# A long two-stage kernel: ten ahead units instead of eight, seven of them in three passes, and late weights loaded one by one

## The chip, the cores and the metric

The kernel runs on one core of a Trainium2 chip. The metric is the device time of one execution in microseconds (us), lower is better. Five things work side by side on the core: TensorE (PE, its weight loads are listed as PEld), VectorE (DVE), ScalarE (ACT), GpSimd (POOL) and the DMA queues, which SyncE (SP) and here and there ACT issue. A program counts its hand-overs with semaphores, and each engine runs its own list in order, so an instruction that waits holds up all that stands behind it on its engine.

## The reference

```python
def _attn_ref(x, filt_r, filt_i):            # x: 2 x 3008 x 256
    X = np.fft.rfft(x, axis=1)
    Y = X * (filt_r + 1j * filt_i)[None, :, :]
    return np.fft.irfft(Y, n=x.shape[1], axis=1).astype(np.float32)

def _moe_ref(x, w_in, w_out, alpha):         # 6016 x 256, w_in 256 x 2048, w_out 2048 x 256
    h = x @ w_in
    g = np.maximum(h, 0.0) + alpha * np.minimum(h, 0.0)
    return (g @ w_out).astype(np.float32)

def _moe2_ref(x, w_in, w_out):
    h = np.maximum(x @ w_in, 0.0)
    return (h * h @ w_out).astype(np.float32)

def reference(**kwargs):
    x = _attn_ref(x, filt_r, filt_i).reshape(B * S, D)
    return _moe2_ref(_moe_ref(x, ...), ...)
```

## The kernel before

**Spectral part.** Each batch element ("first" = b0, "second" = b1) is transformed as a 47 x 64 Fourier transform, all as matrix products. For the second element the first stage is 16 units (`A_UNITS`) of 96 x 512 numbers. One unit is one matmul with the 96 x 96 matrix `const_a1`, a copy of its PSUM bank to SBUF by ACT, and a store to the DRAM tensor `t_rows` by SP. Operands in plain fp32 make two matmul records per unit. Where operands are split in a high and a low part, both of type fp32r, a product is three matmuls, high x high, low x high and high x low, one record each; the feed-forward layers and the spectra of the first element work in that way.

**Slots.** After the first element's spectral part come 192 slots, n = 0 to 191: 12 groups of some 500 tokens, each through 8 pairs of weight tiles p = 0 to 7, for each of the two layers. `up(n)` is 12 matmuls; ACT (`L757`) and DVE (`L945`, `L955`) make the hidden pieces from them; POOL makes two more sums of pieces (`L621` and `L624`, named T2 and T4); ACT rounds seven pieces to `g_hi` (`L633`), DVE forms `g_lo` (`L930`), and two slots later PE does `down_high(n - 2)` (14 matmuls, `L1188` and `L1190`) and `down_low(n - 2)` (7 matmuls, `L1201`). In slots 0 and 1 there is no down part.

**Weights.** A weight pair p is loaded by SP to `w_raw`, four sums of its tiles are made (by five POOL instructions, `L563` to `L569`, for p = 0 to 4, and by four DVE instructions, `L846` to `L853`, for p = 5 to 7, which is `LATE_W` on), ACT rounds it to `w_hi`, and POOL subtracts to `w_lo` (`L553`). `up(p)` of the first group waits for `w_lo`. Pairs 5 to 7 are late because their place in SBUF holds `a_ahead` and `x_ahead` first, the results and inputs of the ahead units.

**Ahead units.** Eight units (`AHEAD_A`) of the second element run before slot 0 (`transform_ahead`, `L1029`): unit 0 before the last inverse of the first element, units 1 to 5 after `y_first(0)`, units 6 and 7 after `y_first(1)`. `y_first(half)` (`L1112`) makes half of group 0 from `vc`, which is the stored result `v_rows` of the first element loaded again. The other eight units (`transform_1`, `L1035`) stand behind slots 0, 1, 2, 2, 3, 3, 4, 4 (`A_SLOT`). SP stores the ahead results two units at a time (`store_ahead`), and loads weight pairs 5, 6 and 7 in one go when all eight are stored (`a_ahead_stored`).

The order on every engine is written out by hand: the blocks `@block.sync`, `@block.gpsimd`, `@block.scalar`, `@block.vector` and `@block.tensor` are the lists of SP, POOL, ACT, DVE and PE.

Of the kernel before, what the change touches and what calls it, by code (L numbers as in the profile page):

```python
# [1383 lines left out]
```

## Time and profile before

| | us |
|---|---|
| median of three runs | 1112.49 |
| lowest and highest | 1112.28, 1113.65 |
| the profiled execution, its own time | 1113.78 |
| span of its instructions | 1112.0 |

The profile page divides the span by engine. PE is busy for 1105.1 us of the span, DVE for 961.0, ACT for 663.8, POOL for 643.8. The busy time of PE is modelled and its matmuls are pipelined, so the start of one matmul and that of the next tell more than the length of either. The chain of work that ended last, followed backwards from the last instruction, is 86% PE. The granted TensorE clock is 1.00 of full speed over the whole span, 2.4 GHz.

### The profile page before, as it was taken

The page shows a single profiled execution, that of the slowest core. Times are in us where ns is not written, and L with a number is a line of the kernel's source. Part 1 is how long each engine was busy: PE and PEld are TensorE (multiplying, and loading weights), DVE is VectorE, ACT ScalarE, POOL GpSimd, SP SyncE. Part 2 cuts the span into 40 slices and gives each one's busy share as a digit, 9 for nine tenths or more (in the row PEclk, how much of TensorE's full clock was granted, in tenths as well). Part 3 has the DMA queues.
Part 4 walks back from the last instruction along what each step waited for, and adds up shares of the span by engine and source line. Part 5 has one row for each costly group of instructions (what it writes and reads, how often), then busy time and mean ns, then how long its engine had stood idle before and what let it go on. Part 6 is the DMA issues. An engine that isn't in the chain of part 4 may idle for free.

```text
span 1112.0 us, 17235 instructions
## 1 busy us (share of the span) xinstructions
PE 1105.1 (99%) x6911; PEld 985.3 (89%) x6911; DVE 961.0 (86%) x1100; ACT 663.8 (60%) x785; POOL 643.8 (58%) x479
## 2 busy tenths in 40 slices
PE   8999999999999999999999999999999999999998
PEld 7568989898999999999999999999999999999998
DVE  4758999999898988888888898888888888888887
ACT  5966667666556555655556656555555555555654
POOL 1836687877566556556557455555555555455453
PEclk9999999999999999999999999999999999999999
DMA  9973325152130421221218510110110110110100
GB/s 251 271 212 88 93 77 155 47 156 61 40 114 1 139 88 52 88 88 52 88 64 314 210 38 1 38 38 1 38 38 1 38 38 1 38 37 1 38 19 20
DMA packets 57865, 88.22 MB, mean 79 GB/s; under 512 B 4920, under 2 KB 45624, under 8 KB 57784
## 3 DMA queue, kind: packets, MB, share of 16 engines
q1 hardware_dynamic: 57584, 86.95, 25.3%
q8 instruction: 55, 0.90, 0.3%
q14 instruction: 26, 0.21, 0.1%
q10 hardware_dynamic: 200, 0.15, 0.0%
HBM read 53.79 MB, written 33.29 MB: 78 GB/s over the span
## 4 chain that ended last, share of the span: by engine, by line
PE 86%; DVE 5%; POOL 3%; issue 2%; ACT 2%; DMA 1%; SPq 0%; ACTq 0%; DVEq 0%; POOLq 0%
PE bank L1156 14%; PE bank L1161 14%; PE bank L1157 14%; PE bank L1190 12%; PE bank L1188 12%; PE bank L1201 12%; PE bank L1133 2%; DVE y_im_b L836 1%; DVE g_lo L930 1%; ACT swapped_b L633 1%; PE bank L1002 1%; DVE g_raw L945 1%; PE bank L1056 1%; PE bank L1058 1%; POOL g_raw L621 1%
## 5 line engine op out<-in xcount | busy, mean ns | idle before, releaser
L621 POOL TENSOR_TENSOR g_raw<-g_raw 128x250 f32<-128x250 f32 (+1 forms) x191 | 272.1, 1425 | 391.8 <-DVE g_raw L955 391.8
L930 DVE TENSOR_TENSOR g_lo<-g_raw,g_hi 128x1750 fp32r<-128x1750 f32 (+1 forms) x191 | 424.6, 2223 | 49.6 <-ACT g_hi L633 48.7
L757 ACT ACTIVATE g_raw<-bank 128x500 f32<-128x500 f32 (+1 forms) x384 | 226.1, 591 | 316.2 <-PE bank L1161 275.7
L633 ACT ACTIVATE g_hi<-g_raw 128x1750 fp32r<-128x1750 f32 (+1 forms) x191 | 318.9, 1670 | 56.9 <-POOL g_raw L624 54.9
L1190 PE MATMUL bank<-g_hi,w_lo 128*128 128x250 f32 (+1 forms) x1337 | 320.2, 279 | 0.0
L1188 PE MATMUL bank<-g_hi,w_hi 128*128 128x250 f32 (+1 forms) x1337 | 319.8, 279 | 0.0
L1156 PE MATMUL bank<-in_hi,w_hi 128*128 128x500 f32 (+1 forms) x768 | 302.3, 394 | 0.0
L1157 PE MATMUL bank<-in_hi,w_lo 128*128 128x500 f32 (+1 forms) x768 | 298.3, 388 | 0.0
L1190 PEld LDWEIGHTS bank<-g_hi,w_lo 128*128 128x128 f32 x1337 | 252.7, 189 | 7.5
L1188 PEld LDWEIGHTS bank<-g_hi,w_hi 128*128 128x128 f32 x1337 | 252.5, 189 | 7.5
L624 POOL TENSOR_TENSOR g_raw<-g_raw 128x250 f32<-128x250 f32 (+1 forms) x191 | 244.7, 1281 | 15.0
L1161 PE MATMUL bank<-in_lo,w_hi 128*128 128x500 f32 (+1 forms) x768 | 236.8, 390 | 0.0
L1201 PE MATMUL bank<-g_lo,w_hi 128*128 128x250 f32 (+1 forms) x1337 | 187.7, 279 | 0.0
L1201 PEld LDWEIGHTS bank<-g_lo,w_hi 128*128 128x128 f32 x1337 | 171.5, 189 | 2.5 <-DVE g_lo L930 0.7
L1161 PEld LDWEIGHTS bank<-in_lo,w_hi 128*128 128x128 f32 x768 | 144.4, 188 | 30.1
L1156 PEld LDWEIGHTS bank<-in_hi,w_hi 128*128 128x128 f32 x768 | 144.6, 188 | 24.4 <-issue 1.6
L1157 PEld LDWEIGHTS bank<-in_hi,w_lo 128*128 128x128 f32 x768 | 144.5, 188 | 23.6 <-issue 1.4
L945 DVE SCALAR_TENSOR_TENSOR g_raw<-g_raw,rest_sb,bank 128x500 f32<-128x500 f32 (+1 forms) x192 | 136.2, 730 | 25.4 <-ACT g_raw L757 25.1
L948 DVE TENSOR_TENSOR g_raw<-g_raw,bank 128x500 f32<-128x500 f32 (+1 forms) x192 | 127.6, 671 | 32.3 <-ACT g_raw L757 31.3
L955 DVE TENSOR_TENSOR g_raw<-g_raw 128x500 f32<-128x500 f32 (+1 forms) x192 | 136.7, 712 | 6.6
L553 POOL TENSOR_TENSOR s_lo<-s_raw,s_hi 128x512 fp32r<-128x512 f32 (+1 forms) x24 | 32.9, 1371 | 1.4 <-DVE in_lo L886 1.4
L553 POOL TENSOR_TENSOR w_lo<-w_raw,w_hi 128x1408 fp32r<-128x1408 f32 x8 | 26.4, 3305 | 7.0 <-ACT w_hi L633 7.0
(91 smaller groups left out, 611.2 us busy)
## 6 DMA issues: line engine op xcount, KB each, us to landing
filt_b<-filt SPq DMA_DIRECT2D x36, 256.0 KB, 4.7
v_rows<-v_out_b SPq DMA_DIRECT2D x24, 256.0 KB, 3.5
vc<-v_rows SPq DMA_DIRECT2D x22, 256.0 KB
w_rows<-s_hi SPq DMA_DIRECT2D x8, 704.0 KB, 3.7
w_rows<-s_lo SPq DMA_DIRECT2D x8, 704.0 KB, 3.2
w_hi<-w_rows SPq DMA_DIRECT2D x8, 704.0 KB, 5.2
w_lo<-w_rows SPq DMA_DIRECT2D x8, 704.0 KB, 7.7
w_raw<-w SPq DMA_DIRECT2D x8, 512.0 KB, 6.1
```

The source lines that it names most:

```text
L621: pool.tensor_tensor(g_raw[:, r, T2, 0:h], g_raw[:, r, B22, 0:h], g_raw[:, r, T1N, 0:h], ALU.add).then_inc(t2_ready, 1)
L624: pool.tensor_tensor(g_raw[:, r, T4, 0:h], g_raw[:, r, B21, 0:h], g_raw[:, r, T2, 0:h], ALU.subtract).then_inc(t4_ready, 1)
L633: return act.activation(dst, src, ACT.Copy)
L757: act.activation(g_raw[:, r, 2 * j:2 * j + 2, 0:h], h_ps[j][:, 0:2 * h].rearrange("p (j d) -> p j d", j=2), ACT.Relu, scale=-1.0 if n < SL ...
L930: dve.tensor_tensor(g_lo[:, q, B11:T4 + 1, 0:h], g_raw[:, q, B11:T4 + 1, 0:h], g_hi[:, q, :, 0:h], ALU.subtract).then_inc(g_lo_ready, 1)
L945: dve.scalar_tensor_tensor(out=piece, in0=piece, scalar=rest_sb[:, f:f + 1], in1=hidden, op0=ALU.mult, op1=ALU.add).then_inc(g_ready, 1)
L1156: pe.matmul(o, w_hi[:, p, 2 * j + k, :], in_hi[:, g % 2, k, cols], start=(k == 0), stop=False)
L1157: pe.matmul(o, w_lo[:, p, 2 * j + k, :], in_hi[:, g % 2, k, cols], start=False, stop=False)
L1161: mm = pe.matmul(o, w_hi[:, p, 2 * j + k, :], in_lo[:, g % 2, k, cols], start=False, stop=(k == KD - 1))
L1188: pe.matmul(o, w_hi[:, p, tile, :], g_hi[:, q, piece - B11, 0:h], start=(first and (side == 0 or g == LAST_G and b == 3)), stop=False, ski ...
L1190: pe.matmul(o, w_lo[:, p, tile, :], g_hi[:, q, piece - B11, 0:h], start=False, stop=False, skip_group_check=True)
L1201: mm = pe.matmul(o, w_hi[:, p, tile, :], g_lo[:, q, piece, 0:h], start=False, stop=(last or final and b < 3), skip_group_check=True)
```

## The change

Ten units run ahead instead of eight, and six stay behind slots: 0, 1, 2, 2, 3, 3. Unit 0 stays as it was. Units 1 to 7 all stand between `y_first(0)` and `y_first(1)` and go in three passes: `x_ahead` is rounded to `x_hi` (units 1 and 2 by POOL, 3 to 7 by ACT), DVE subtracts in place to `x_lo`, and the matrix comes in split form too (`a1_parts`, cast by POOL from a `const_a1` load that is three times as wide). Units 8 and 9 are in plain fp32 after `y_first(1)`, from the ordinary buffers `x_raw`. Two more PSUM banks, 4 and 5, take ahead units, and so `up(0)` waits for the copy of unit 5. SP issues the loads of units 8 and 9 ahead of the last store of `v_rows`. Weight pair 5 is loaded as soon as the first four ahead units are stored, 6 and 7 after the rest, and the sums of pair 5 move from DVE in slot 2 to POOL ahead of slot 0; those of pairs 6 and 7 are on DVE in slots 2 and 3 instead of 3 and 4.

```diff
-AHEAD_BANK = (2, 3, 0, 1)
-AHEAD_PART = (1, AHEAD_A - 2, AHEAD_A)
-A_SLOT = [None] * AHEAD_A + [0, 1, 2, 2, 3, 3, 4, 4]
+AHEAD_ALL = AHEAD_A + 2
+AHEAD_BANK = (2, 3, 0, 1, 4, 5)
+AHEAD_PART = (1, AHEAD_A, AHEAD_ALL)
+A_SLOT = [None] * AHEAD_ALL + [0, 1, 2, 2, 3, 3]
...
+LATE_SUMS = LATE_W + 1
...
@@ block.sync @@
             for n in range(B_UNITS):
+                if n == B_UNITS - 1:
+                    for u in range(AHEAD_A, AHEAD_ALL):
+                        load_x(u)
                 store_v(f0, *divmod(n, B_HALF), n % f0.vs)
...
+            def load_late(p):
+
+                for j in IN_PLACE[p - LATE_W]:
+                    sp.wait_ge(a_ahead_stored[j], 32)
+                load_w1(p)
+
             store_ahead(0)
-            for u in range(AHEAD_A, AHEAD_A + f1.xs):
+            store_ahead(2)
+            for u in range(AHEAD_ALL, AHEAD_A + f1.xs):
                 load_x(u)
-            for u in range(2, AHEAD_A, 2):
-                store_ahead(u)
-            sp.wait_ge(a_ahead_stored, 16 * AHEAD_A)
-            for p in range(LATE_W, FP):
-                load_w1(p)
+            store_ahead(4)
+            load_late(LATE_W)
+            store_ahead(6)
+            for u in range(AHEAD_A, AHEAD_ALL):
+                load_x(u + f1.xs)
+            for u in range(AHEAD_A, AHEAD_ALL):
+                store_t(f1, u, u % f1.outs)
+            for p in range(LATE_W + 1, FP):
+                load_late(p)
@@ block.gpsimd @@
             for p in range(LATE_W):
                 if p + 1 < LATE_W:
                     w_sums(p + 1)
+                else:
+
+                    pool.wait_ge(const_a1_loaded, 16)
+                    pool.tensor_copy(a1_parts[:, :], const_a1_sb[:, ROWS:3 * ROWS]).then_inc(a1_parts_ready, 1)
+                    x_high(1)
+                    x_high(2)
                 w_low(p)
...
             for s in f0.v_stored:
                 pool.wait_ge(s, 16 * (B_UNITS // f0.vs + 1))
+
+            w_sums(LATE_W)
@@ block.scalar @@
+                if n == B_UNITS - 1:
+                    x_high(3)
...
             for u in range(AHEAD_PART[0]):
                 ahead_copy(u)
+            x_high(4)
             v_copy(f0, B_UNITS - 1, (B_UNITS - 1) // f0.vs, (B_UNITS - 1) % f0.vs, (B_UNITS - 1) % 2)
+            x_high(5)
...
             in_high(0, (0,))
+            x_high(6)
+            x_high(7)
             act.wait_ge(f0.v_stored[(B_UNITS - 1) % f0.vs], 48)
@@ block.vector @@
+            for u in range(1, 6):
+                x_low(u)
             in_low(0, (0,))
+            for u in range(6, AHEAD_A):
+                x_low(u)
...
-                if LATE_W <= n + 3 < FP:
-                    w_sums(n + 3)
+                if LATE_SUMS <= n + 4 < FP:
+                    w_sums(n + 4)
@@ block.tensor @@
+                if 0 < u < AHEAD_A:
+                    pe.wait_ge(a1_parts_ready, 1)
+
+                    pe.wait_ge(x_lo_ready, u)
+                    pe.matmul(ps, a1_parts[:, 0:ROWS], x_hi[:, u - 1, :], start=True, stop=False)
+                    pe.matmul(ps, a1_parts[:, ROWS:2 * ROWS], x_hi[:, u - 1, :], start=False, stop=False)
+                    pe.matmul(ps, a1_parts[:, 0:ROWS], x_lo[:, u, :], start=False, stop=True).then_inc(f1.a_done, 1)
+                    return
```

On PE, between the two halves of `y_first`, three rows stood before, of which the middle one is ahead units 1 to 5 (two records each):

```order
L1112 MATMUL bank<-const_y_sb,vc 128x34
L1029 MATMUL bank<-x_ahead,const_a 96x512 x5
L1112 MATMUL bank<-const_y_sb,vc 128x94 x5
L1112 MATMUL bank<-const_y_sb,vc 128x34
L1029 MATMUL bank<-x_ahead,const_a 96x512 x2
L1156 MATMUL bank<-in_hi,w_hi 128x504
```

After the change, the end of that stretch reads (the first three rows here are the last of seven such triples):

```order
L1105 MATMUL bank<-x_hi,a_parts 96x512
L1106 MATMUL bank<-x_hi,a_parts 96x512
L1107 MATMUL bank<-x_lo,a_parts 96x512
L1197 MATMUL bank<-const_y_sb,vc 128x94 x5
L1197 MATMUL bank<-const_y_sb,vc 128x34
L1114 MATMUL bank<-x_raw_b,const_a 96x512 x2
L1241 MATMUL bank<-in_hi,w_hi 128x504
```

Two units in fp32 still stand behind `y_first(1)`, now units 8 and 9, and the seven in three passes all stand ahead of it.

On POOL, the passage from the weights of the first slots to the first T2 and T4 (`L621`, `L624`) was:

```order
L569 TENSOR_TENSOR w_raw<-w_raw 128x128
L553 TENSOR_TENSOR w_lo<-w_raw,w_hi 128x1408 x2
L621 TENSOR_TENSOR g_raw<-g_raw 128x252
L624 TENSOR_TENSOR g_raw<-g_raw 128x252
L621 TENSOR_TENSOR g_raw<-g_raw 128x252
```

and is now:

```order
L588 TENSOR_TENSOR w_lo<-w_raw,w_hi 128x1408
L617 CAST a_parts<-const_a 96x192
L608 CAST x_hi<-x_ahead 96x512 x2
L588 TENSOR_TENSOR w_lo<-w_raw,w_hi 128x1408
L598 TENSOR_TENSOR w_raw<-w_raw 128x128
L600 TENSOR_SCALAR w_raw<-w_raw 128x128
L601 TENSOR_TENSOR w_raw<-w_raw 128x128
L602 TENSOR_TENSOR w_raw<-w_raw 128x128
L604 TENSOR_TENSOR w_raw<-w_raw 128x128
L668 TENSOR_TENSOR g_raw<-g_raw 128x252
L671 TENSOR_TENSOR g_raw<-g_raw 128x252
```

The five rows from `L598` on are the sums of pair 5; they wait for its load, and slot 0's T2 and T4 (`L668`, `L671`) stand behind them.

On SP, with what each waits for, the stores of the ahead units and the late weights stood so:

```order
L339 DMA t_rows<-a_ahead 48x8x128 [waits a_out_ready_b1]
L339 DMA t_rows<-a_ahead 48x8x128
L327 DMA x_raw_b<-x 96x512 x4
L339 DMA t_rows<-a_ahead 48x8x128 [waits a_out_ready_b1]
L339 DMA t_rows<-a_ahead 48x8x128
L339 DMA t_rows<-a_ahead 48x8x128 [waits a_out_ready_b1]
L339 DMA t_rows<-a_ahead 48x8x128
L339 DMA t_rows<-a_ahead 48x8x128 [waits a_out_ready_b1]
L339 DMA t_rows<-a_ahead 48x8x128
L380 DMA w_raw<-w 128x1024 [waits a_ahead_stored]
L380 DMA w_raw<-w 128x1024 x2
```

and now:

```order
L359 DMA t_rows<-a_ahead 48x8x128 [waits a_out_ready_b1]
L359 DMA t_rows<-a_ahead 48x8x128
L359 DMA t_rows<-a_ahead 48x8x128 [waits a_out_ready_b1]
L359 DMA t_rows<-a_ahead 48x8x128
L347 DMA x_raw_b<-x 96x512 x2
L359 DMA t_rows<-a_ahead 48x8x128 [waits a_out_ready_b1]
L359 DMA t_rows<-a_ahead 48x8x128
L400 DMA w_raw<-w 128x1024 [waits a_ahead_stored1,a_ahead_stored0]
L359 DMA t_rows<-a_ahead 48x8x128 [waits a_out_ready_b1]
L359 DMA t_rows<-a_ahead 48x8x128
```

The load of pair 5 (`L400`) now waits for the first two pairs of stores, with the third issued ahead of it and the fourth behind it.

## Rows read from the trace of the kernel before

**Rows 1.** The page: busy time (share) and instructions of PE, and the chain by engine

```profile
PE 1105.1 (99%) x6911; PEld 985.3 (89%) x6911; DVE 961.0 (86%) x1100; ACT 663.8 (60%) x785; POOL 643.8 (58%) x479
...
PE 86%; DVE 5%; POOL 3%; issue 2%; ACT 2%; DMA 1%; SPq 0%; ACTq 0%; DVEq 0%; POOLq 0%
```

**Rows 2.** The chain in order of time, 55 to 80: start us, us, what

```profile
55.99 2.43 DMA v_rows<-v_out_b
...
59.05 2.08 DMA vc<-v_rows
61.26 1.50 PE bank L1112 x12
...
64.53 0.23 PE bank L1156
...
74.48 0.12 PE bank L1188
...
76.12 0.81 PE bank L1201 x7
76.93 1.72 PE bank L1035 x4
```

**Rows 3.** Timeline of PE, 45.1 to 46: start us, us, engine line op tiles shape

```profile
45.14 0.39 PE L1044 MATMUL bank<-t_hi_b,const 128*128 128x512 f32 x1
45.37 0.40 PE L1046 MATMUL bank<-t_lo_b,const 128*128 128x512 f32 x1
45.61 0.59 PE L1056 MATMUL bank<-y_re_b,const_full 128*128 128x512 f32 x1
```

**Rows 4.** Timeline of ACT, 40 to 105

```profile
56.63 0.59 ACT L633 ACTIVATE in_hi<-bank 128x504 fp32r<-128x504 f32 x1 [0.66 <-PE bank L1112]
...
59.34 2.54 ACT L633 ACTIVATE a_ahead<-bank 96x512 f32<-96x512 f32 x5 [2.12 <-PE bank L1029]
...
71.40 1.67 ACT L633 ACTIVATE g_hi<-g_raw 128x1764 fp32r<-128x1764 f32 x1
```

**Rows 5.** Timeline of DVE, 45 to 105

```profile
57.32 0.68 DVE L886 TENSOR_TENSOR in_lo<-bank,in_hi 128x504 fp32r<-128x504 f32 x1 [4.52 <-ACT in_hi L633]
...
72.31 0.69 DVE L955 TENSOR_TENSOR g_raw<-g_raw 128x504 f32<-128x504 f32 x1
73.10 2.56 DVE L930 TENSOR_TENSOR g_lo<-g_raw,g_hi 128x1764 fp32r<-128x1764 f32 x1
...
92.47 0.28 DVE L846 SCALAR_TENSOR_TENSOR w_raw<-w_raw 128x128 f32<-128x128 f32 x1
...
94.38 1.98 DVE L930 TENSOR_TENSOR g_lo<-g_raw,g_hi 128x1764 fp32r<-128x1764 f32 x1
```

**Rows 6.** Timeline of POOL, 20 to 110

```profile
22.58 0.46 POOL L563 TENSOR_TENSOR w_raw<-w_raw 128x128 f32<-128x128 f32 x1 [22.16 <-DMA w_raw<-w]
...
24.57 0.46 POOL L569 TENSOR_TENSOR w_raw<-w_raw 128x128 f32<-128x128 f32 x1
...
69.55 0.74 POOL L621 TENSOR_TENSOR g_raw<-g_raw 128x252 f32<-128x252 f32 x1 [14.78 <-DVE g_raw L955]
70.37 0.73 POOL L624 TENSOR_TENSOR g_raw<-g_raw 128x252 f32<-128x252 f32 x1
...
73.89 2.37 POOL L624 TENSOR_TENSOR g_raw<-g_raw 128x252 f32<-128x252 f32 x1
```

**Rows 7.** Timeline of SP's queue, 0 to 130

```profile
59.96 0.82 SPq L339 DMA_DIRECT2D t_rows<-a_ahead  x2
```

**Rows 8.** Tile a_ahead: the eight stores of SP, issue to landing

```profile
DMA to landing us min/median/max: 2.6/3.7/4.1
```

**Rows 9.** Tile w_raw, 55 to 110: the three late loads, issue to landing

```profile
DMA to landing us min/median/max: 3.6/4.5/6.6
```

**Rows 10.** Busy times of 61 to 70.5; the last number is GB/s moved

```profile
61.00:70.50 9.50, 9.33 (x43) 6.78 (x43) 3.18 (x5) 5.04 (x9) 0.87 (x2) 1.00 0.90 245
```

**Rows 11.** Timeline of PE, 96.6 to 97.4

```profile
96.71 0.86 PE L1201 MATMUL bank<-g_lo,w_hi 128*128 128x252 f32 x6
```

More of the change, by code:

```diff
@@ L92 @@
 LATE_W = 5
+LATE_SUMS = LATE_W + 1
+IN_PLACE = [range(p * W_T * P // (2 * COLS), min(AHEAD_A // 2, -(-(p + 1) * W_T * P // (2 * COLS))))
+            for p in range(FP - LATE_W)]
 W2_SLOT = [38, 45, 51, 58, 66, 74, 82, 90]
 W2_LOW = ((3, 0, 4), (4, 4, 8), (5, 8, W_T))
+X_PLACE = 17 * P
 WARM_COLS, WARM_X = 2 * P, 3
@@ L282, in spectral_mix_two_ffn @@
         x_ahead_loaded = [sem(f"x_ahead_loaded{n}") for n in range(AHEAD_A // 2)]
-        a_ahead_stored = sem("a_ahead_stored")
+        a_ahead_stored = [sem(f"a_ahead_stored{n}") for n in range(AHEAD_A // 2)]
+        a1_parts_ready = sem("a1_parts_ready")
+        x_hi_pool, x_hi_act, x_lo_ready = sem("x_hi_pool"), sem("x_hi_act"), sem("x_lo_ready")
         y_done = sem("y_done")
@@ L469, in _ @@
                 if n < SLOTS_1:
-                    for u in range(AHEAD_A, A_UNITS):
+                    for u in range(AHEAD_ALL, A_UNITS):
                         if A_SLOT[u] == n and u + f1.xs < A_UNITS:
                             load_x(u + f1.xs)
-                    for u in range(AHEAD_A, A_UNITS):
+                    for u in range(AHEAD_ALL, A_UNITS):
                         if A_SLOT[u] + 1 == n:
@@ L481, in _ @@
                             if u == 0:
-                                sp.wait_ge(a_ahead_stored, 16 * AHEAD_A)
+                                for stored in a_ahead_stored:
+                                    sp.wait_ge(stored, 32)
                                 for s in f1.a_stored:
@@ L677, in ahead_copy, with x_high @@
                 act.wait_ge(f1.a_done, done(u))
-                copy(a_ahead[:, u, :], m_ps[AHEAD_BANK[u % 4]][0:ROWS, :]).then_inc(f1.a_out_ready, 1)
+                copy(a_ahead[:, u, :] if u < AHEAD_A else f1.a_out[:, u % f1.outs, :],
+                     bank[AHEAD_BANK[u % len(AHEAD_BANK)]][0:ROWS, :]).then_inc(f1.a_out_ready, 1)
+            def x_high(u):
+                act.wait_ge(x_ahead_loaded[u // 2], 16)
+                copy(x_hi[:, u - 1, :], x_ahead[:, u, :]).then_inc(x_hi_act, 1)
             for u in range(0, TURN_UNIT, 2):
@@ L733, in _ @@
                 if n < SLOTS_1:
-                    for u in range(AHEAD_A, A_UNITS):
+                    for u in range(AHEAD_ALL, A_UNITS):
                         if A_SLOT[u] + 1 == n:
@@ L855, in w_sums @@
             def w_sums(p):
-                sums(w_raw[:, p, :, :], w_loaded[p], 16, (w_sums_ready, w_sum_step), p - LATE_W)
+                sums(w_raw[:, p, :, :], w_loaded[p], 16, (w_sums_ready, w_sum_step), p - LATE_SUMS)
             def t_low(n):
@@ L887, in in_low, with x_low @@
                                       in_hi[:, g % 2, half, 0:2 * HALF[k]], ALU.subtract).then_inc(in_lo_ready, 1)
+            def x_low(u):
+                if u < 3:
+                    dve.wait_ge(x_hi_pool, u)
+                else:
+                    dve.wait_ge(x_hi_act, u - 2)
+                dve.tensor_tensor(x_lo[:, u, :], x_ahead[:, u, :], x_hi[:, u - 1, :], ALU.subtract
+                                  ).then_inc(x_lo_ready, 1)
+            for u in range(1, 6):
+                x_low(u)
             in_low(0, (0,))
+            for u in range(6, AHEAD_A):
+                x_low(u)
             for s in f0.v_stored:
@@ L1214, in _ @@
             pe.wait_ge(f0.v_ready, done(B_UNITS - 1))
+            pe.wait_ge(f1.a_out_ready, done(len(AHEAD_BANK) - 1))
             for n in range(2 * SLOTS_1):
@@ L1218, in _ @@
                 if n == LAG:
-                    pe.wait_ge(f1.a_out_ready, done(AHEAD_A - 1))
+                    pe.wait_ge(f1.a_out_ready, done(AHEAD_ALL - 1))
                 if n >= LAG:
@@ L1232, in _ @@
                     ys = sum(FP * k + Y_P < n for k in range(GROUPS - 1))
-                    for u in range(AHEAD_A, A_UNITS):
+                    for u in range(AHEAD_ALL, A_UNITS):
                         if A_SLOT[u] == n:
```

51 lines of the change are left out of this document (34 added, 17 removed).

## The prediction, made before the changed kernel ran

> **What bounds the kernel now.** I read the page first, for the share of each engine and the chain by engine [rows 1]. PE is busy for 99% of the span and carries 86% of the chain; no other engine carries more than 5%. So a microsecond of matmul that disappears is a microsecond of time, unless a wait takes its place, and a wait that is added on PE costs its full length. Next I read the chain in order of time over the stretch that is changed [rows 2], to get the moments at which PE reaches each step: the last store of v_rows is issued at 55.99 and lands at 58.42, the reloaded vc arrives at 61.1, y_first(1) begins at 61.26, slot 0 at 64.53, down_high(0) at 74.48, down_low(0) at 76.12, and two fp32 units behind a slot take 1.72. Then I read the timelines of the other engines over the same stretch, to see how long before each of these moments its inputs are ready [rows 4 to 7], and the landing times and the rate of the DMAs [rows 8 to 10].
>
> **Three passes instead of fp32.** A fp32 unit costs 1.72 / 2 = 0.86 us of PE [rows 2]. Three passes over 512 columns are not in the trace on 96 rows, but they are on 128: successive starts are 0.23 and 0.24 apart [rows 3], so one unit is 3 x 0.235 = 0.70 us. Seven units save 7 x 0.16 = 1.1 us.
>
> **The order around y_first(1).** y_first(0) is done at 56.57, just before ACT's copy starts at 56.63 [rows 4]. Before, five units follow: 56.57 + 5 x 0.86 = 60.87, and PE stands idle until 61.26, 0.39 us. Now seven short units follow: 56.57 + 7 x 0.705 = 61.50. vc is there by then, so y_first(1) begins 0.24 later than before, and since two fp32 units still follow, slot 0 does too. Behind slot 4 two units of 0.86 are gone. Ahead of any new wait the sum is +0.24 - 1.72 = **-1.48 us**, of which 1.1 is the cheaper product and 0.39 the idle time filled.
>
> **Preparing the operands.** This I cost at nothing, and the cover is idle time. ACT's five roundings of 512 columns take a pitch of 0.49 us each (five copies in 2.54, [rows 4]). It has 0.66 idle before 56.63 and 2.12 before 59.34, and the two roundings that stand in the latter take 1.0; the other three stand at steps where it waits for PE. DVE's x_low are 512 columns wide, like its 0.68 us in_low, and it stands idle for 4.52 us before 57.32 [rows 5]; five of them take about 3.1 and the last two come after 57.9, while PE needs unit 6 at 60.1. POOL's two casts of 512 columns and one of 192 have no row; twice its 0.74 for 252 columns gives 1.5 each, some 3.6 in all, before a w_lo that slot 4 first needs. POOL does nothing at all for 14.78 us before 69.55 [rows 6]. If this cover failed, each 1 us of lateness in x_lo would delay PE by up to 1 us. ACT's copies of units 1 to 5 run from 59.34 to 61.88, ahead of the moments at which units 7, 8 and 9 and slot 0 need their banks.
>
> **Loads ahead of the last v_rows store.** Units 8 and 9 bring 0.39 MB that now stands ahead of that store. At 245 GB/s [rows 10] it occupies the queue for 1.6 us. SP issues it when the store before has been issued, so most of it should be through before 57, when the data of the store at 55.99 begins to move. I take 0; the upper bound is 1.6 less PE's new slack of 0.4, 1.2 us.
>
> **The sums of pair 5.** Here the change adds a wait. POOL's five sums wait for the load of pair 5, and behind them on POOL are T2(0) and T4(0); behind T4(0) ACT's g_hi(0), behind it DVE's g_lo(0), and PE's down(0) needs both. Let L be the landing of that load. The sums take 22.58 to 25.03, 2.45 us [rows 6], T2 and T4 from 69.55 to 71.10, 1.55, g_hi 1.68 [rows 4], g_lo 1.98 when alone [rows 5]; with four hand-overs of about 0.06 that is L + 7.9. PE now wants g_lo(0) at 76.12 + 0.24 = 76.36. So the wait is free up to L = 68.5, and above that PE loses L - 68.5.
>
> When is L? SP may issue the load when the first four units are stored. The copy of unit 3 ends at 59.34 + 0.59 + 2 x 0.49 = 60.9 [rows 4]; SP is free then (it ends its first two stores at 60.78, [rows 7]), so the second two stores are issued at 60.95 and 61.4. Stores land 2.6 to 4.1 after issue, the median is 3.7 [rows 8], so the load is issued between 64.0 and 65.5, likely at 65.0. A late load took 3.6 when the queue was empty and up to 6.6 behind others [rows 9]. That bounds L by 64.0 + 3.6 = 67.6 and 65.5 + 6.6 = 72.1. To choose, I count bytes from 61.0, when the data of the first store begins to move: six stores and two x loads of 0.197 MB, and 0.524 MB of weights, 2.1 MB in all. At 245 GB/s this takes 8.6 us, and a landing comes about 0.4 after the last byte: 70.0. With an empty queue it would be 65.0 + 3.6 = 68.6. Between the two I take L = 69.5, nearer to the count, since four DMAs do stand in the queue ahead of this load, and the new wait as 69.5 - 68.5 = **+1.0 us**.
>
> **POOL against DVE.** T4 took 0.73 alone but 2.37 at 73.89, while g_lo was running on DVE [rows 5, 6]: one engine holds the other up. With L = 69.5, T2(0) and T4(0) fall on 72.0 to 73.6, where DVE has its L955 of 0.69 at 72.31. Neither may touch the other, or T4(0) may come 0.7 later; the bounds are 0 and +0.7. I take **+0.2**, as a short overlap is nearer to the short row. The Trainium skill, page "SBUF — State Buffer", section "SBUF: two separate sides", says that a DVE instruction with two SBUF inputs and a GpSimd instruction share one port pair as an exclusive lock, held for the whole instruction by whichever starts first. By that rule the full 0.7 falls due and the sum ends at +0.2 instead of -0.3; the row at 73.89 agrees with it in kind.
>
> **Late weights otherwise.** Before, DVE makes pair 7's sums from 92.47 to 94.38 and g_lo(3) after them, done at 96.36, while PE starts down_low(3) at 96.71 [rows 5, 11]. With two units gone PE would want it at 96.71 - 1.48 = 95.2, a stall of 1.1. But DVE's sums are gone from slot 4, which is 1.9 us, and that leaves 0.8 to spare. So this edit gives no time itself; it keeps the 1.72 from being given back.
>
> **The sum.** -1.48 + 1.0 + 0.2 = **-0.3 us**. The profiled execution (1113.78, span 1112.0) would be at 1113.5, and since the median of the runs shown is 1.29 less than the profiled one, I forecast a median of 1112.49 - 0.3 = **1112.2 us**. A measurement of this kernel can tell some 0.2% from no change, 2.2 us; this forecast is "the same".
>
> **Rivals.**
> 1. **The load of pair 5 is early.** If L is 68.5 or less, POOL is never late and the whole -1.48 stays: 1111.0. For it: an empty queue gives 67.6 to 69.1. Against: two x loads and two stores are in the queue ahead of it. The Trainium skill, page "DMA: Bandwidth & Descriptors", section "Anatomy of one DMA — SWDGE (gpsimd) path", fits one DMA by a fixed 2.0 us and its bytes at 436 GB/s; that makes 3.2 us for this load and so this case, against 3.6 in the emptiest row here.
> 2. **The load of pair 5 is late, and the kernel slower.** The mechanism is the same chain on POOL, and it turns the sign from L = 69.8 on. At L = 71 the stall is 2.5, and -1.48 + 2.5 + 0.2 = +1.2 gives 1113.7; at the bound of 72.1 it is 3.6, and with the contention at 0.2 or 0.7 the net is +2.3 or +2.8: 1114.8 to 1115.3. The largest landing times in the rows speak for it; against it, that 6.6 belongs to a load with two others of its size ahead.
> 3. **The vc path is late.** The two x loads push the last store back by up to the bound of 1.2: 1112.2 + 1.2 = 1113.4. ACT's copies of units 1 to 5 stand behind that store too.
> 4. **The change doesn't bring its gain**, because the x_lo aren't there when PE is, or three passes on 96 rows are no cheaper than fp32: then 1.1 is missing: 1113.3.
>
> **Chances.** The forecast case (L from 68.6 to 70.3) 50%, rival 1 20%, rival 2 18%, rivals 3 and 4 5% each, and 2% for something faster than all of this. For 8 in 10 the range goes from 1110.8, the full gain with the usual scatter of the runs, to 1114.0, rival 2 up to L of 71.3. The chance of faster by over 0.2% (below 1110.3) is 0.04, since no case gives it without scatter; slower by over 0.2% (above 1114.7) needs rival 2 near its bound or with rival 3, 0.07; within, 0.89, which holds nearly all of every case.
>
> **What would show it.** In the profile after: triples on PE with starts 0.235 apart and y_first(1) at 61.5 without idle; POOL's first sum with an idle time ended by the DMA of w_raw, near 69.5, and T2(0) near 72 instead of 69.55; PE idle, or in the chain DVE's g_lo, ahead of down_low(0) at about 77.5; slot 5's down_low(3) at about 96.4 instead of 96.71. The forecast is wrong if POOL's first sum starts before 68.5 or after 70.5, or if a wait shows anywhere else on PE before slot 8.

## The result, and the profile after

The changed kernel takes 1120.09 us (median of 6 runs, 1118.78 to 1120.61) against 1113.62 for the kernel before on the same chip (6 runs, 1112.28 to 1114.29): a ratio of 1.0059, interval 1.0046 to 1.0072. It is slower by 0.6%, where -0.3 us was forecast; the range ended at 1114.0. The profiled execution took 1119.06, with a span of 1117.1, so it is 5.3 us above the profiled one of before, and its span is 5.1 longer.

From the profile page after, the same two rows as in [rows 1]: busy time by engine, then the chain by engine.

```profile
PE 1106.6 (99%) x6918; PEld 988.1 (88%) x6918; DVE 971.9 (87%) x1103; ACT 666.8 (60%) x790; POOL 646.8 (58%) x487
...
PE 83%; DVE 6%; POOL 4%; issue 2%; ACT 2%; DMA 2%; SPq 1%; ACTq 0%; DVEq 0%; POOLq 0%
```

PE fell from 86% to 83% of the chain, and DVE, POOL and DMA rose by a point each. To see where, I cut both traces where the first product with `w_lo` of each slot starts (us, worked out from the starts of PE's rows; "to slot 0" is counted from the last inverse of the first element, since the start-up before it scatters):

| kernel | to slot 0 | 0 to 2 | 2 to 3 | 3 to 4 | 4 to 5 | 5 to 6 | 0 to 6 | 6 to 40 |
|---|---|---|---|---|---|---|---|---|
| before | 10.71 | 7.20 | 6.93 | 6.92 | 6.92 | 7.52 | 35.49 | 203.70 |
| after | 10.73 | 7.20 | 9.80 | 10.20 | 5.79 | 7.54 | 40.53 | 203.74 |

All of the 5 us lies in slots 2, 3 and 4: +2.9 and +3.3 in two of them, and in slot 4 only 1.1 is gained where two units are gone that took 1.72 together. From slot 6 on nothing differs. PE's waits between 55 and 106, all that there are (engine, tile and line waiting, what released it, us in total, times, longest):

```profile
PE bank L1273 <- ACT g_hi L680: 2.3, 1, 2.3
PE bank L1286 <- DVE g_lo L1001: 1.7, 1, 1.7
```

The first was in the forecast; the second was not. The chain after, in order of time, leads through both of these, ACT's `g_hi` and DVE's `g_lo` (the view of [rows 2]):

```profile
61.77 3.49 DMA t_rows<-a_ahead
65.33 5.12 DMA w_raw<-w
70.60 0.46 POOL w_raw L598
...
73.39 0.70 POOL g_raw L668
74.16 0.72 POOL g_raw L671
74.91 1.68 ACT g_hi L680
76.61 2.00 DVE g_lo L1001
78.61 1.31 DVE g_raw L1016 x2
79.94 0.68 DVE g_raw L1026
80.63 0.21 DVE w_raw L904
...
82.52 4.96 DVE g_lo L1001
87.53 1.08 PE bank L1286 x7
88.61 2.90 PE bank L1120 x4
```

Down to 76.61 this is rival 2's chain. Then it doesn't return to PE: DVE works without a gap until 87.5, and one `g_lo` takes 5.0 us. The timelines of POOL and DVE, 82 to 99, with the idle time of POOL at 70.60 ahead:

```profile
70.60 0.45 POOL L598 TENSOR_TENSOR w_raw<-w_raw 128x128 f32<-128x128 f32 x1 [15.91 <-DMA w_raw<-w]
...
82.34 3.27 POOL L588 TENSOR_TENSOR w_lo<-w_raw,w_hi 128x1408 fp32r<-128x1408 f32 x1
...
91.19 3.27 POOL L588 TENSOR_TENSOR w_lo<-w_raw,w_hi 128x1408 fp32r<-128x1408 f32 x1
```

```profile
82.45 5.03 DVE L1001 TENSOR_TENSOR g_lo<-g_raw,g_hi 128x1764 fp32r<-128x1764 f32 x1
...
91.29 5.01 DVE L1001 TENSOR_TENSOR g_lo<-g_raw,g_hi 128x1764 fp32r<-128x1764 f32 x1
...
98.24 1.99 DVE L1001 TENSOR_TENSOR g_lo<-g_raw,g_hi 128x1764 fp32r<-128x1764 f32 x1
```

Twice POOL's `w_lo` begins 0.1 us ahead of `g_lo`. `g_lo` stands until it is done and then takes its own time: 82.34 + 3.27 + 1.98 = 87.6, and the row ends at 87.5. Before, `w_lo` waited for a `w_hi` that ACT made from DVE's sums of the same slot. From the trace of the kernel before, DVE, ACT and POOL:

```profile
79.50 1.98 DVE L930 TENSOR_TENSOR g_lo<-g_raw,g_hi 128x1764 fp32r<-128x1764 f32 x1
...
79.61 1.39 ACT L633 ACTIVATE w_hi<-w_raw 128x1408 fp32r<-128x1408 f32 x1 [1.64 <-DVE w_raw L853]
...
81.07 3.50 POOL L553 TENSOR_TENSOR w_lo<-w_raw,w_hi 128x1408 fp32r<-128x1408 f32 x1 [1.65 <-ACT w_hi L633]
```

So `w_lo` began when `g_lo` was under way, and `g_lo` kept its 1.98; POOL, which had time, was the one to wait. With the sums a slot earlier `w_hi` is ready long before, and POOL comes first.

The granted clock (the last number but two of the row) shows one thing more:

```profile
89.00:92.40 3.40, 3.40 (x7) 1.58 (x6) 3.33 (x6) 1.18 (x2) 2.75 (x3) 0.50 0.25 57
```

After the second stall the clock is at 0.50 of full speed, 1.2 GHz, for 3.4 us, and at 1.00 from 76 to 89 and from 92.4 to 98. Theory A, then: two losses, POOL's late chain in slot 2 and the order of `w_lo` and `g_lo` in slots 3 and 4, each enough by itself to undo the gain. Theory B: it is one loss, the late load, and the rest (the second stall, the clock) only follows from it. Theory C: a good part is the clock. In the recorded expectations the second half of A is called the lock theory and B the late-load theory.

### The profile page after: what moved, and what is told of

Same layout as the page of the kernel before. It is cut to its first block, busy times and chain, and to the rows that moved or that the text cites. A ratio compares the mean times of both kernels' runs of the same rounds, so it can differ in the third digit from the quotient of the medians.

```text
span 1117.1 us, 17269 instructions
## 1 busy us (share of the span) xinstructions
PE 1106.6 (99%) x6918; PEld 988.1 (88%) x6918; DVE 971.9 (87%) x1103; ACT 666.8 (60%) x790; POOL 646.8 (58%) x487
## 4 chain that ended last, share of the span: by engine, by line
PE 83%; DVE 6%; POOL 4%; issue 2%; ACT 2%; DMA 2%; SPq 1%; ACTq 0%; DVEq 0%; POOLq 0%
PE bank L1241 14%; PE bank L1246 14%; PE bank L1242 13%; PE bank L1286 12%; PE bank L1275 12%; PE bank L1273 12%; DVE g_lo L1001 2%; PE bank L1218 2%; DVE y_im_b L894 1%; ACT swapped_b L680 1%; DVE g_raw L1016 1%; POOL y_re_b L626 1%; PE bank L1141 1%; PE bank L1143 1%; POOL g_raw L668 1%
## 5 line engine op out<-in xcount | busy, mean ns | idle before, releaser
L668 POOL TENSOR_TENSOR g_raw<-g_raw 128x250 f32<-128x250 f32 (+1 forms) x191 | 273.9, 1434 | 384.1 <-DVE g_raw L1026 384.1
L1001 DVE TENSOR_TENSOR g_lo<-g_raw,g_hi 128x1750 fp32r<-128x1750 f32 (+1 forms) x191 | 429.9, 2251 | 53.2 <-ACT g_hi L680 52.4
L671 POOL TENSOR_TENSOR g_raw<-g_raw 128x250 f32<-128x250 f32 (+1 forms) x191 | 242.9, 1272 | 15.0
L1016 DVE SCALAR_TENSOR_TENSOR g_raw<-g_raw,rest_sb,bank 128x500 f32<-128x500 f32 (+1 forms) x192 | 136.2, 730 | 22.2 <-ACT g_raw L815 21.9
L1026 DVE TENSOR_TENSOR g_raw<-g_raw 128x500 f32<-128x500 f32 (+1 forms) x192 | 138.2, 720 | 6.6
L680 ACT ACTIVATE ct<-bank 128x250 f32<-128x250 f32 (+1 forms) x24 | 9.1, 380 | 29.9 <-PE bank L1286 29.9
```

What stands on the lines that cost most here:

```text
L668: pool.tensor_tensor(g_raw[:, r, T2, 0:h], g_raw[:, r, B22, 0:h], g_raw[:, r, T1N, 0:h], ALU.add).then_inc(t2_ready, 1)
L671: pool.tensor_tensor(g_raw[:, r, T4, 0:h], g_raw[:, r, B21, 0:h], g_raw[:, r, T2, 0:h], ALU.subtract).then_inc(t4_ready, 1)
L680: return act.activation(dst, src, ACT.Copy)
L1001: dve.tensor_tensor(g_lo[:, q, B11:T4 + 1, 0:h], g_raw[:, q, B11:T4 + 1, 0:h], g_hi[:, q, :, 0:h], ALU.subtract).then_inc(g_lo_ready, 1)
L1016: dve.scalar_tensor_tensor(out=piece, in0=piece, scalar=rest_sb[:, f:f + 1], in1=hidden, op0=ALU.mult, op1=ALU.add).then_inc(g_ready, 1)
```

## The experiments

Each is compared with the kernel before on the same chip. The stretches, cut as above, are those of the one profiled execution:

| kernel | to slot 0 | 2 to 3 | 3 to 4 | 4 to 5 | 5 to 6 | 0 to 6 |
|---|---|---|---|---|---|---|
| e1 sums back | 10.83 | 6.93 | 6.92 | 5.47 | 8.83 | 35.36 |
| e2 POOL's sums later | 10.84 | 6.93 | 6.92 | 8.43 | 7.52 | 37.00 |
| e3 w_lo waits | 10.77 | 11.68 | 6.92 | 5.20 | 7.54 | 38.55 |
| e4 both | 10.71 | 6.93 | 6.92 | 5.40 | 8.12 | 34.57 |
| e5 cut in three, on e2 | 10.71 | 6.93 | 6.92 | 6.56 | 7.54 | 35.16 |
| e6 load first | 10.88 | 10.54 | 6.92 | 5.20 | 7.54 | 37.41 |
| e7 plain fp32 | 11.87 | 6.93 | 6.92 | 5.43 | 8.10 | 34.58 |
| e8 warm | 10.72 | 10.44 | 8.86 | 7.13 | 7.51 | 41.17 |
| e9 cut in three, on e4 | 11.00 | 6.93 | 6.92 | 5.45 | 8.24 | 34.74 |
| e10 cut in three, on e1 | 10.70 | 6.93 | 6.92 | 5.72 | 9.11 | 35.89 |
| e11 weights alone | 10.97 | 13.94 | 6.92 | 8.43 | 7.52 | 44.02 |

**The two causes apart, and together.** The first undoes the sums alone: DVE makes those of pair 5 too, in slots 2, 3 and 4 as before.

```diff
-LATE_SUMS = LATE_W + 1
+LATE_SUMS = LATE_W
...
-            w_sums(LATE_W)
...
-                if LATE_SUMS <= n + 4 < FP:
-                    w_sums(n + 4)
+                if LATE_SUMS <= n + 3 < FP:
+                    w_sums(n + 3)
```

> The change with one part undone: the sums of pair 5 are back on DVE in slot 2, those of 6 and 7 in slots 3 and 4; ten units ahead, three passes and the one-by-one loads stay. Two theories on the 5.1 us that the changed kernel's span is longer. Lock theory: the sums one slot sooner let POOL's w_lo start together with DVE's g_lo, which then takes 5.0 instead of 2.0 us, twice. Late-load theory: the loss comes from T2(0) and T4(0) waiting for the load of pair 5 (it lands at 70.4), and what follows is only its echo. This kernel takes away both, so both expect no stall in slots 2 and 3 and g_lo at 2.0 to 2.6 us. The order theory of the prediction says that down_low(3) then stalls about 1.1 us in slot 5. Both: 1.5 to 0.4 us faster than before. If it is still over 3 us slower than before, both are wrong and the cause lies in the ten units or in the loads.

Measured: 1113.66 against 1113.62, ratio 0.9998 (0.9989 to 1.0008). PE's waits from 76 to 106, and `g_lo` and `w_lo` of slot 2:

```profile
PE bank L1284 <- DVE g_lo L999: 1.0, 1, 1.0
...
78.68 1.98 DVE L999 TENSOR_TENSOR g_lo<-g_raw,g_hi 128x1764 fp32r<-128x1764 f32 x1
...
80.26 3.50 POOL L588 TENSOR_TENSOR w_lo<-w_raw,w_hi 128x1408 fp32r<-128x1408 f32 x1 [1.64 <-ACT w_hi L678]
```

The order of before is back: POOL stands for 1.64 us until ACT has `w_hi`, and starts behind `g_lo`. The whole loss is gone with the sums. A gain of 0.4 to 1.5 us was expected and none is measured: of the 1.72 that two units took, 1.3 is given back in slot 5, at the one wait left, and 0.3 in slot 4.

The second keeps the new division of the sums, but POOL makes those of pair 5 behind slot 1's T4 instead of ahead of slot 0's:

```diff
-            w_sums(LATE_W)
...
                 pool.tensor_tensor(g_raw[:, r, T4, 0:h], ...).then_inc(t4_ready, 1)
+                if n == 1:
+                    w_sums(LATE_W)
```

> The change with POOL's sums of pair 5 moved from ahead of slot 0 to behind slot 1's T4. T2(0) and T4(0) no longer wait for the load; the sums of all late pairs still come a slot sooner than before. Late-load theory: both stalls go, the kernel is 1.0 to 1.5 us faster than before. Lock theory: the stall in slot 2 goes (2.7 us), but w_lo and g_lo still start together in slots 3 and 4, with g_lo near 5 us, so that the kernel stays 1 to 3 us slower than before.

Measured: 1116.9, ratio 1.0024 (1.0013 to 1.0035), 3.3 us slower than before by the medians, where the lock theory had 1 to 3. The wait in slot 2 is gone and one collision of `w_lo` and `g_lo` is left. POOL's `w_lo`, DVE's `g_lo`, and PE behind it:

```profile
87.91 3.26 POOL L588 TENSOR_TENSOR w_lo<-w_raw,w_hi 128x1408 fp32r<-128x1408 f32 x1
...
88.02 5.01 DVE L1001 TENSOR_TENSOR g_lo<-g_raw,g_hi 128x1764 fp32r<-128x1764 f32 x1
...
93.08 1.08 PE L1286 MATMUL bank<-g_lo,w_hi 128*128 128x252 f32 x7 [2.96 <-DVE g_lo L1001]
```

Nothing waits for the late load here, and still there is a `g_lo` of 5.01: the collision doesn't follow from it. In the profiled execution the clock is at 1.00 throughout these slots; what the other runs add is under "The clock".

The third leaves the sums where the change put them and makes the late `w_lo` wait for DVE's `g_lo` of the slot:

```diff
                 if LATE_W <= n + 2 < FP:
+                    pool.wait_ge(g_lo_ready, n - 1)
                     w_low(n + 2)
```

> The change with one wait more on POOL: w_lo of pairs 5 to 7 waits until DVE has done the g_lo of two slots back, so that the two don't start together. The wait for the late load stays. Lock theory: g_lo is back at 2.0 to 2.6 us, the stall of 1.8 us in slot 3 and the time at a lower granted clock behind it go, and the kernel is 0.5 to 2 us slower than before instead of 6.5, that is by the stall in slot 2 less the gain. Late-load theory: nothing changes against the changed kernel, or it gets slower by the added wait.

Measured: 1116.96, ratio 1.0035 (1.0022 to 1.0048). DVE and POOL:

```profile
82.90 1.98 DVE L1002 TENSOR_TENSOR g_lo<-g_raw,g_hi 128x1764 fp32r<-128x1764 f32 x1
...
84.96 3.25 POOL L588 TENSOR_TENSOR w_lo<-w_raw,w_hi 128x1408 fp32r<-128x1408 f32 x1 [2.13 <-DVE g_lo L1002]
```

PE has one wait left, for `g_hi` in slot 2, and after it 3 us at half clock (the second row):

```profile
PE bank L1274 <- ACT g_hi L681: 3.0, 1, 3.0
...
78.00:81.00 3.00, 3.00 (x16) 3.00 (x15) 2.96 (x4) 3.00 (x4) 0.00 (x0) 0.50 0.39 97
```

A wait of `w_lo` that POOL can afford gives back all of slots 3 and 4; it does nothing for slot 2. The kernel was expected to be 0.5 to 2 us slower than before and is 3.3 slower by the medians: the half clock, which was to go with the stall in slot 3, now stands behind the one in slot 2.

The fourth has both edits.

> Both edits together: POOL's sums of pair 5 behind slot 1's T4, and w_lo of the late pairs behind g_lo of two slots back. If the two costs are separate and add up, this kernel is 0.5 to 1.5 us faster than before, and PE has no idle time over 0.3 us between slot 0 and slot 6. The wait can push w_lo onto DVE's next instruction with two inputs in SBUF (L1026), by up to 1.7 us per slot; if that costs as much as the collision with g_lo, the kernel is 0 to 2 us slower than before.

Measured: 1113.01, ratio 0.9993 (0.9983 to 1.0003), the profiled span 1111.2. PE waits once, and `w_lo` again comes behind `g_lo`. The last row is the DVE instruction that it meets instead:

```profile
PE bank L1287 <- DVE g_lo L1002: 0.3, 1, 0.3
...
87.82 1.98 DVE L1002 TENSOR_TENSOR g_lo<-g_raw,g_hi 128x1764 fp32r<-128x1764 f32 x1
...
89.89 3.24 POOL L588 TENSOR_TENSOR w_lo<-w_raw,w_hi 128x1408 fp32r<-128x1408 f32 x1 [2.13 <-DVE g_lo L1002]
...
91.14 2.53 DVE L1027 TENSOR_TENSOR g_raw<-g_raw 128x504 f32<-128x504 f32 x1
```

Theory A holds: slots 0 to 6 take 40.53 with both faults, 38.55 or 37.00 with one, 34.57 with neither, 0.9 less than before. The order isn't free, though: `L1027` takes 0.68 elsewhere and 2.53 behind `w_lo`, 1.9 us more, where `g_lo` lost 3.0. Of the 1.72 that two units took, 0.2 and 0.6 are still lost in slots 4 and 5. This is the best version found, and it can't be told from the kernel before.

**The weight part by itself.** This is the kernel before with the new order of late weights alone: eight ahead units in fp32, pair 5 loaded early, its sums on POOL, the others a slot earlier.

```diff
-            for u in range(2, AHEAD_A, 2):
-                store_ahead(u)
-            sp.wait_ge(a_ahead_stored, 16 * AHEAD_A)
-            for p in range(LATE_W, FP):
-                load_w1(p)
+            store_ahead(2)
+            store_ahead(4)
+            load_late(LATE_W)
+            store_ahead(6)
+            for p in range(LATE_W + 1, FP):
+                load_late(p)
...
+            w_sums(LATE_W)
...
-                if LATE_W <= n + 3 < FP:
-                    w_sums(n + 3)
+                if LATE_SUMS <= n + 4 < FP:
+                    w_sums(n + 4)
```

> The kernel before with the weight part of the change alone: eight units ahead in fp32 as before, pair 5 loaded after the first four stores, its sums on POOL ahead of slot 0, those of 6 and 7 a slot sooner. Here four x loads stand ahead of the stores, so the load of pair 5 lands at 71 to 72. If the weight part carries the whole loss, this kernel is 4 to 6 us slower than before: the stall in slot 2 is 3 to 4 us, and DVE's chain after it (8.85 us per slot with a g_lo of 5 us) lags PE by less than in the changed kernel, since PE has 1.7 us more work of its own in slot 4. If the loss needs the ten units as well, it is under 2 us slower.

Measured: 1122.2, ratio 1.0074 (1.0059 to 1.009), where 4 to 6 us slower was expected and 8.7 is measured. PE's waits, a `g_lo`, and the clock behind the first wait:

```profile
PE bank L1200 <- ACT g_hi L645: 4.1, 1, 4.1
PE bank L1213 <- DVE g_lo L942: 1.2, 1, 1.2
...
92.49 5.02 DVE L942 TENSOR_TENSOR g_lo<-g_raw,g_hi 128x1764 fp32r<-128x1764 f32 x1
...
77.00:83.50 6.50, 5.55 (x23) 5.01 (x24) 5.56 (x8) 5.08 (x6) 2.07 (x3) 0.50 0.25 72
```

The weight part brings the loss without the unit part. How large it is can't be set against the change, because the load is later here. In this kernel four x loads stand on SP ahead of the second pair of stores, from 59.84 to 62.54, so the load is issued at 67.58 and lands at 71.84, 1.4 later than in the change and 2.0 later counted from slot 0. Slot 2 is 7.0 us longer than before; 4.1 of that is the wait, and behind it the clock is at half for 6.5 us.

**The unit part by itself.** e4 with units 1 to 7 in plain fp32 and without casts, `x_lo` and split matrix:

```diff
-                if 0 < u < AHEAD_A:
+                if False:
```

> The kernel with both edits (sums behind slot 1's T4, w_lo waits for g_lo), but units 1 to 7 in plain fp32: no rounding to x_hi, no x_lo, two matmul records per unit. If three passes save 0.16 us per unit, y_first(1) begins 1.1 to 1.2 us later against y_first(0), and the kernel is 1.1 us slower than the one with both edits, that is 0.5 us slower than before. If the time goes elsewhere on the way (the stalls in slots 4 and 5 shrink by the same amount because DVE's chain gets a head start), it is less than 0.5 us slower than the one with both edits.

Measured: 1114.97, ratio 1.001 (1.0001 to 1.0019). The stretch to slot 0 is 11.87 instead of e4's 10.71. Three passes are worth 1.16 us, where 1.1 was worked out. From slot 0 to 6 the two kernels are alike (34.58 and 34.57). By the medians this one is 1.3 us slower than before (0.1 to 2.1 by the interval), where 0.5 was expected.

**The load in front of the third stores.** To see whether the stores ahead of it make it late, e3 with these two exchanged on SP:

```diff
-            store_ahead(4)
             load_late(LATE_W)
+            store_ahead(4)
```

> POOL's sums of pair 5 ahead of slot 0 as in the changed kernel, w_lo waits for g_lo (no collision), and the stores of ahead units 4 and 5 moved behind the load of pair 5 on SP. With these stores ahead of it the load landed at 70.8 and PE stood 3.1 us in slot 2. If the queue ahead of the load sets L, 0.39 MB less brings L down by 1.4 to 1.6 us and the stall to about 1.6 us: 1.5 us faster than without the move, and 1.7 more if the granted clock then no longer falls. If the load's own latency sets L, nothing changes.

Measured: 1115.22, ratio 1.0017 (1.0008 to 1.0026). It is issued at 65.65 and lands at 69.80, 4.15 us, against 65.58 and 70.79, 5.21 us, in e3. Two stores ahead of it cost 1.06 us of landing, and PE's wait falls from 3.0 to 1.8, where 1.4 to 1.6 less landing and a wait of 1.6 were expected:

```profile
PE bank L1274 <- ACT g_hi L681: 1.8, 1, 1.8
```

In the profiled execution slot 2 still is 3.6 us longer than before, the stall and the half clock after it together. That execution took 1117.39, 2.2 above the median. The load can't be brought early enough in this way.

**The clock.** The changed kernel with five spare matmuls ahead of `down_high(0)`, whose result nobody reads:

```diff
                     pe.wait_ge(f1.a_out_ready, done(AHEAD_ALL - 1))
+                    keep_warm(5, m_ps[3])
                 if n >= LAG:
                     down_high(n - LAG)
```

> The changed kernel with five matmuls on zeros (256 columns, 2.1 us in all) on PE ahead of down_high(0), inside its stall of 2.5 us; nothing else waits for them. The stalls stay as they are, by both theories. Clock theory A: the fall of the granted clock to 0.5 for 3.4 us near slot 4 comes from the two stalls taken together; with one filled it doesn't come, and the kernel is 1.5 to 2 us faster than the changed one. Theory B: the second stall (1.8 us, slot 3) alone brings it; no change.

Measured: 1119.64, ratio 1.0055 (1.0042 to 1.0069), as slow as the change within both intervals. The fall of the clock stayed away, as one theory had it, and the 1.5 to 2 us that it was to bring didn't come. The clock was 1.00 throughout, but PE waits twice for `g_lo`:

```profile
89.00:92.40 3.40, 3.25 (x14) 2.11 (x15) 3.30 (x8) 1.32 (x3) 1.13 (x2) 1.00 0.00 0
...
89.15 1.07 PE L1286 MATMUL bank<-g_lo,w_hi 128*128 128x252 f32 x7 [1.67 <-DVE g_lo L1001]
...
98.01 1.08 PE L1286 MATMUL bank<-g_lo,w_hi 128*128 128x252 f32 x7 [1.67 <-DVE g_lo L1001]
```

Theory C falls for the change: slots 3 and 4 together take 15.99 in both. (Slot 2 is 0.6 longer here; the load of pair 5 lands 0.5 later, counted from slot 0.) The two waits are 8.86 apart, and that is DVE's work of one slot: `g_lo` 5.0, two `L1016` 1.4, `L1026` 0.7, four sums 1.9, with short overlaps in the rows. In the change DVE keeps the same beat (its `g_lo` start at 82.45 and 91.29), so what half clock takes from PE between them it would otherwise have waited.

Where DVE doesn't set the beat, the half clock lies on the path. In e3, slot 2 is 1.9 us longer than in the change, of which 0.7 is the longer wait (3.0 against 2.3). In the profiled execution of e6, slot 2 is 3.6 longer than before and 1.8 of it is the wait; the rest falls in the stretch at half clock. The other runs of e6 agree: six of ten have a mean granted clock of 1.00 and spans of 1112.5 to 1113.2, four (the profiled one among them) have 0.998 and 1113.8 to 1115.6, on average 1.6 us more. In e2, two of seven have 0.999 and 1113.1 and 1113.7, five have 0.998 or 0.997 and 1114.6 to 1116.9. That would be why e2 is 3.3 us slower than before by its median, and only 1.5 in slots 0 to 6 of its profiled execution, which has no half clock there. It isn't shown by an edit: none kept the clock up in e2, e3 or e6, and the runs without a trace may also differ in how long PE waited.

**Shorter holds.** Three runs cut the late `w_lo` into pieces of 512, 512 and 384 columns, so that `g_lo` might slip in between: on e2 (e5), on e4 (e9) and on e1 (e10).

```diff
+LOW_PARTS = ((0, 4), (4, 8), (8, W_T))
...
-                low(w_lo[:, p, :, :], w_raw[:, p, :, :], w_hi[:, p, :, :], w_lo_ready)
+                for a, b in ((0, W_T),) if p < LATE_W else LOW_PARTS:
+                    low(w_lo[:, p, a:b, :], w_raw[:, p, a:b, :], w_hi[:, p, a:b, :], w_lo_ready)
```

> POOL's sums of pair 5 behind slot 1's T4, no added wait, but the w_lo of pairs 5 to 7 cut into three instructions of 512, 512 and 384 columns instead of one of 1408. Lock theory: the two engines hold each other up for one whole instruction of the other, so g_lo can be late by 1.2 us at most instead of 3.2, less than DVE's slack of about 1.2; no stall on PE over 0.3 us between slot 0 and slot 6, and 1.2 to 1.7 us faster than before. If instead both share a rate, or the bytes that POOL moves are what counts, the cut changes nothing: g_lo stays near 5 us and the kernel is 2 to 3 us slower than before, as with one instruction.

> All three remedies on the ten units: POOL's sums of pair 5 behind slot 1's T4, w_lo of the late pairs waits for g_lo of two slots back, and it is cut in three. With the wait but uncut, PE still stood 0.7 us in slots 4 and 5, since w_lo fell on DVE's L1026 (2.6 us instead of 0.7). Cut, L1026 can be late by 1.2 us at most. If the holds by whole instructions are the whole cost, slots 0 to 6 take 33.8 us (35.5 before, 34.6 uncut) and the kernel is 1.3 to 1.7 us faster than before. If each further POOL instruction starts ahead of a waiting DVE one, the cut gives nothing and it stays at 34.6.

> The late sums on DVE as before the change (slots 2, 3, 4), ten units, and w_lo of the late pairs cut in three. Uncut, this kernel equals before: 1.7 us of matmuls gone, 1.3 us of it given back as a stall in slot 5. If that stall comes from w_lo holding up DVE's L1024 (1.2 us instead of 0.7 in slots 3 and 4, 2.2 in slot 5), the cut takes away about half of it: 0.5 to 0.8 us faster than before. If it comes from the circle of DVE's sums, ACT's rounding and the next relu, as the prediction's 1.1 us assumed, the cut changes nothing: within 0.3 us of before.

Measured: e5 1113.46, ratio 0.9996 (0.9988 to 1.0005); e9 1113.05, 0.9997 (0.9988 to 1.0006); e10 1113.78, 1.0002 (0.9993 to 1.0011). In e5, POOL and DVE meet as in e2:

```profile
86.98 5.32 POOL L589 TENSOR_TENSOR w_lo<-w_raw,w_hi 128x512 fp32r<-128x512 f32 x3
...
87.09 3.08 DVE L1003 TENSOR_TENSOR g_lo<-g_raw,g_hi 128x1764 fp32r<-128x1764 f32 x1
```

`g_lo` takes 3.08 instead of 5.01: it waits for the first piece (1.33 us) and then goes ahead of the second, which needs 3.05. So the hold is by instruction, and not a shared rate. A gain of 1.2 to 1.7 us on before and no stall over 0.3 was expected; the loss of e2 is gone, but PE still waits 1.1 us for `g_lo` in slot 4, and the time is that of before.

Beside the wait of e4 the cut adds nothing: slots 0 to 6 take 34.74 in e9, where 33.8 was expected if it worked. DVE is held twice there, by 1.2 us in `L1029` and by 0.8 in the next `g_lo`, as much as the one hold of 1.9 in e4. In e10 the cut does nothing either: PE waits 1.3 and 0.3 us, for DVE's `g_lo` and for `L1016`.

## Why the prediction was wrong, point by point

**Three passes, the order around y_first(1), preparing the operands: right in what they cost.** The triples start 0.235 apart and y_first(1) follows them without idle (PE after; the view of [rows 3]):

```profile
59.85 0.40 PE L1105 MATMUL bank<-x_hi,a_parts 96*96 96x512 f32 x1
60.09 0.39 PE L1106 MATMUL bank<-x_hi,a_parts 96*96 96x512 f32 x1
60.32 0.39 PE L1107 MATMUL bank<-x_lo,a_parts 96*96 96x512 f32 x1
...
61.24 1.45 PE L1197 MATMUL bank<-const_y_sb,vc 96*128 96x94 f32 x12
```

The way to slot 0 grew by 0.02 instead of 0.24. POOL's two casts took 1.17 together, where 1.5 each was allowed. DVE's first five `x_low` took 5.03 instead of 3.1, and the two after them 1.27. POOL's `w_lo` and DVE's `x_lo` after the change:

```profile
51.52 3.17 POOL L588 TENSOR_TENSOR w_lo<-w_raw,w_hi 128x1408 fp32r<-128x1408 f32 x1
...
52.62 5.03 DVE L953 TENSOR_TENSOR x_lo<-x_ahead,x_hi 96x512 fp32r<-96x512 f32 x5
...
58.17 1.27 DVE L953 TENSOR_TENSOR x_lo<-x_ahead,x_hi 96x512 fp32r<-96x512 f32 x2
```

The first of the five stands until `w_lo` ends at 54.69 and takes 2.62 us; the other four start 0.60 apart. That is the collision of slots 3 and 4 once more, and here DVE's idle time of 4.5 us covered it.

**Loads ahead of the last v_rows store: right at 0.** The store took 2.39 us from issue to landing, 2.43 before. Rivals 3 and 4 are out.

**The sums of pair 5: right in kind, 1.7 us short.** The load was issued at 65.33 (65.0 forecast) and took 5.12 (4.5 taken, 3.6 to 6.6 as bounds): L = 70.45 instead of 69.5. The fit of a fixed 2.0 us and 436 GB/s that rival 1 drew from the Trainium skill, page "DMA: Bandwidth & Descriptors", section "Anatomy of one DMA — SWDGE (gpsimd) path", gives an estimate of 3.2 for it. That fit is for DMAs issued by GpSimd, and this load is SP's; the measured 5.12 decides, and even ahead of the third pair of stores it was 4.15 (e6). From L to `down_low(0)` it was 8.2 us against 7.9 + 0.2. Slot 2 grew by 2.9, where 1.0 + 0.2 was forecast. Of the 1.7 between, 0.95 is the later L, 0.1 the chain, and 0.3 that slot 0 came no later than before and so PE was there sooner. Another 0.16 is that the forecast took PE's demand from the chain, 76.12, while PE's row of `down_low(0)` before starts at 75.96, and 0.1 that PE restarts slower after the wait (from `down_low(0)` to the next row 0.92 instead of 0.81). By itself this is rival 2, and with L = 70.45 its sum gives -1.48 + 1.95 + 0.2 = +0.7 us. No rival reached what was measured; the bound of rival 2 was 1115.3.

**Late weights otherwise: the step that failed.** "DVE's sums are gone from slot 4, which is 1.9 us, and that leaves 0.8 to spare. So this edit gives no time itself" counted the instructions that DVE loses, and not what else their place decides. The sums fed ACT's `w_hi`, and that held POOL's `w_lo` back behind `g_lo`. Without that, POOL goes first, and `g_lo` takes 5.0 instead of 2.0, in two slots: 2 x 3.0 us on the engine that has 0.8 to spare. Slots 0 to 6 take 2.4 us more in e2, which has one such meeting and no wait for the late load, than in e4 (37.00 against 34.57), and 4.0 more in e3, which has the late load and no meeting. The prediction's own sign for this was "a wait shows anywhere else on PE before slot 8"; it stands at 87.5.

The tools for it were in the prediction. It used the row of T4, 2.37 instead of 0.73 [rows 6], and the rule of the Trainium skill, page "SBUF — State Buffer", section "SBUF: two separate sides", for T2 and T4 of slot 0 alone. The runs agree with that rule to some 0.1 us: a `g_lo` that starts 0.1 behind a `w_lo` should last 3.27 + 1.98 - 0.1 = 5.15 and takes 5.0, and behind a piece of 1.33 it should last 3.2 and takes 3.08. The term left out was the longest POOL instruction of the stretch against the longest of DVE, which the change moved relative to each other.

**The stall that was worked out for the case without the moved sums was nearly right**: 1.1 forecast, 1.0 in the waits of e1, where slot 5 is 1.3 longer and slot 4 loses 0.3. So the weight part could save 1.6 us at most, and where it has neither fault it saves 0.8 (slots 0 to 6: 35.36 in e1, 34.57 in e4).

**The sum again, from slots 0 to 6:** +2.9 in slot 2, +3.3 in slot 3, +0.6 in slot 4 beside the units that are gone, -1.7 for these: +5.0, which is what the table shows (40.53 less 35.49) and all but 0.3 of the difference of the profiled executions. The medians are 6.5 apart; the runs of one kernel scatter by up to 2 us, and what the profiled ones don't show of that I can't divide up.

## What to carry over

When a change moves the producer of an instruction on one engine, ask which instruction of another engine it now meets, and which of the two starts first: of two that exclude each other the second pays the whole length of the first, and it should be the one with slack. A wait on the slack engine (here one `wait_ge`, e3 and e4) fixes the order, but look at what it then meets: here an instruction that lost 1.9 us instead of one that lost 3.0. Before work is put ahead of others on a queue, take the load it waits for at its slow bound: a stall that turns the sign 0.3 us above the forecast value is the likeliest way to lose.
